# Attention inside a fused kernel: exponentials kept in PSUM, halves split before the transpose, one product for a pair's sinks

## The chip, the cores and the metric

The kernel runs on one core of a Trainium2 chip. The metric is the device time of one execution in microseconds; the time before is the median of three executions. One further execution was profiled, and all rows below come from it. PE is the matrix engine (PEld its weight loads), DVE the vector engine, ACT the scalar engine, POOL the general one, SP the engine whose queue issues most transfers.

## What is computed

Three stages, one after the other in the reference:

```python
# q, k, v: 4 batches, 8 heads, 768 positions, 64 wide; 4 sink keys, window of 128 keys
scores = scale * q @ k.T
scores = where(is_sink | in_window, scores, -1e9)
a = exp(scores - max(scores)); a = a / (sum(a) + 1e-9)
x = a @ v                                  # reshaped to 3072 tokens x 512
h = x @ w_in; x2 = (h - tanh(h)) @ w_out   # 512 -> 2048 -> 512
logits = x2 @ w_gate + modality_bias[id]   # 8 experts, the best one for each token
out = gate * (relu(x2 @ w1[e]) @ w2[e])    # only the chosen expert
```

## The kernel before

**Tiling.** The 3072 tokens are eight chunks of 384 tokens, three tiles of 128 each. Attention is cut into 192 units: a unit is one head and one tile of 128 queries, and its keys are at most 260 columns: the 128 of the tile before, 4 sinks, and the 128 of its own tile (132 columns where there is no tile before). Six units (two heads, three tiles) are a pair, so a chunk has four pairs, and there are 32 in all. Every product of 32-bit numbers is done as three products of 16-bit halves (low by high, high by low, high by high).

**A unit's way through the engines.** `scores` (L530): two products into a PSUM bank; DVE adds the mask and writes the negated result to `probs` in SBUF (L552) with the row's extreme; ACT takes the exponential from `probs` to `probs` (L557) and sums the row. `normalise` (L562): two tiny DVE operations invert the sum, and ACT writes `normed`, 128 by 260 numbers of 32 bits (L575). `transpose_probs` (L600): PE turns the two blocks of 128 columns (L611) into one of two PSUM banks used in turn, `pt_ps`; ACT copies them out as 16-bit high halves (L594), and DVE subtracts these from the PSUM to get the low halves (L598). Once a pair, DVE gathers the sink columns of six units (L586), PE turns them in three transposes (L625), and ACT and DVE split them in the same way. `weigh_values` (L629) multiplies the halves with those of the values; in a pair's last unit three more products of 384 columns weigh the sinks (L665). `split_x` (L676) copies the finished 384 columns out.

**Order of the work.** The order on each engine is written by hand. The first 28 units run by themselves (`alone`, L1191), beside the conversion of the weights. The others run inside the next chunk products: a `window` (L1208) is one chunk's 16 blocks of the 512-2048-512 stage, in 32 slots. An even slot holds the 12 products of 384 columns of `mlp_in` (L706) for the next block, an odd slot the 9 of 512 columns of `mlp_out` (L762). The slots of a list called `rest` have no unit; from the second window on these are 1, 4, 6, 7, 19, 20, 22 and 26. In a slot with unit n, PE does two thirds of the block's products, then

```python
stage(scores, E, eng, n)
stage(transposes, E, eng, n - 2)
```

then the remaining third, then `weigh_values` of unit n - 3. ACT's order in an even slot is: transposed halves of n - 2, `tanh` of the block (L718), `normalise` of n - 1, exponential of n. In an odd slot `mlp_split` (L737) stands in the place of `tanh`. DVE's order is: (odd slots) `mlp_gate` (L727); inversion of n - 1; mask of n; low halves of n - 2; (odd slots) `mlp_rest` (L747).

**The gate's products.** From the second window on, the chunk before is gated: `gate_slot` (L894), called ahead of everything else in a slot, puts on PE four transposes at slots 5, 11 and 17 (L796), the products for the logits at 7, 13 and 19 (L811), and two ranking products at 25 (L862). In windows 0, 2 and 4 a small product (`spread`, L311) stands at the head of slot 9. All of them borrow the bank of the scores, `s_ps`. Whoever writes to that bank first waits for whoever read it last (`claim_scores`, L670): after a unit's scores the reader is DVE's mask operation, which signals `shifted`.

**After attention.** In the last window the first expert's weights are loaded and prepared, and the experts' products follow.

## Time and profile before

| | |
|---|---|
| median of 3 runs | 1141.67 us (1139.27 to 1142.0) |
| the profiled execution's own time | 1141.86 us |
| its span | 1140.2 us |
| mean granted PE clock | 0.972 |
| units alone | about 15 to 92 us |
| windows 0 to 6, with units | about 92 to 735 us |
| window 7, then experts | 735 to 1140 us |

The span is the profile's first instruction to the last; the time holds 1.7 us more around it. Busy shares are averages over these stretches, and are read stretch by stretch.

### The profile page before, as it was taken

The page shows a single profiled execution, that of the slowest core. Times are in us where ns is not written, and L with a number is a line of the kernel's source. Part 1 is how long each engine was busy: PE and PEld are TensorE (multiplying, and loading weights), DVE is VectorE, ACT ScalarE, POOL GpSimd, SP SyncE. Part 2 cuts the span into 40 slices and gives each one's busy share as a digit, 9 for nine tenths or more (in the row PEclk, how much of TensorE's full clock was granted, in tenths as well). Part 3 has the DMA queues.
Part 4 walks back from the last instruction along what each step waited for, and adds up shares of the span by engine and source line. Part 5 has one row for each costly group of instructions (what it writes and reads, how often), then busy time and mean ns, then how long its engine had stood idle before and what let it go on. Part 6 is the DMA issues. An engine that isn't in the chain of part 4 may idle for free.

```text
span 1140.2 us, 24342 instructions
## 1 busy us (share of the span) xinstructions
PE 1017.1 (89%) x7840; PEld 664.2 (58%) x7840; DVE 729.6 (64%) x2388; ACT 618.5 (54%) x1421; POOL 397.3 (35%) x457
## 2 busy tenths in 40 slices
PE   1657888999999999999999999998896999789997
PEld 0534555565665665566566566654664677567774
DVE  6787978677977867887867876547563333443331
ACT  2675877575766766667666667445322222332221
POOL 3786876222345312325412321110122222122222
PEclk9976999999999999999999999999998999889999
DMA  9832111231212322311231130050023111001111
GB/s 284 282 97 53 34 34 34 75 109 34 61 37 63 62 90 58 69 35 34 38 90 34 34 61 2 1 203 2 29 79 136 43 46 56 28 23 52 46 46 45
DMA packets 24427, 75.14 MB, mean 66 GB/s; under 512 B 9680, under 2 KB 9808, under 8 KB 22800
## 3 DMA queue, kind: packets, MB, share of 16 engines
q1 hardware_dynamic: 15440, 60.58, 19.9%
q0 software_dynamic: 5728, 13.43, 3.8%
q8 instruction: 44, 0.72, 0.3%
q14 instruction: 47, 0.39, 0.1%
q10 hardware_dynamic: 3168, 0.02, 0.1%
HBM read 60.16 MB, written 14.12 MB: 65 GB/s over the span
## 4 chain that ended last, share of the span: by engine, by line
PE 67%; DVE 15%; ACT 6%; issue 6%; POOL 2%; DMA 2%; DVEq 0%; ACTq 0%; SPq 0%; POOLq 0%
PE h_ps L706 16%; PE acc L762 14%; PE pt_ps L1766 11%; PE h_ps L1817 6%; PE acc L1817 5%; PE x_out L665 4%; PE s_ps L542 2%; PE pt_ps L611 2%; DVE g_raw L727 2%; DVE qk_top L385 2%; DVE qk_exp L394 1%; PE s_ps L811 1%; DVE ew_lo L1478 1%; DVE g_lo L747 1%; ACT probs L557 1%
## 5 line engine op out<-in xcount | busy, mean ns | idle before, releaser
L762 PE MATMUL acc<-w_out_all,g_hi 128*128 128x512 f16 x768 | 228.3, 379 | 0.0
L706 PE MATMUL h_ps<-xt_hi,w_in_all 128*128 128x384 f16 x1024 | 211.1, 329 | 16.9 <-DVE g_raw L727 16.8
L762 PE MATMUL acc<-w_out_all,g_lo 128*128 128x512 f16 x384 | 145.4, 379 | 2.5 <-POOL w_out_all L350 1.2
L594 ACT ACTIVATE pt_hi<-pt_ps 128x256 f16<-128x256 f32 (+2 forms) x224 | 83.6, 380 | 110.0 <-PE pt_ps L611 106.0
L706 PEld LDWEIGHTS h_ps<-xt_hi,w_in_all 128*128 128x128 f16 x1024 | 97.6, 99 | 78.2 <-DVE g_raw L727 16.3
L98 POOL TENSOR_TENSOR tick<-tick 1x1 f32<-1x1 f32 x83 | 15.3, 184 | 313.0 <-ACT y L1833 97.8
L747 DVE SCALAR_TENSOR_TENSOR g_lo<-g_raw,batch_scale,g_hi 128x384 f16<-128x384 f32 x128 | 95.2, 743 | 33.1 <-ACT g_hi L737 30.7
L762 PEld LDWEIGHTS acc<-w_out_all,g_hi 128*128 128x128 f16 x768 | 75.0, 98 | 69.2
L598 DVE TENSOR_TENSOR pt_lo<-pt_ps,pt_hi 128x256 f16<-128x256 f32 (+2 forms) x224 | 94.3, 423 | 29.9 <-ACT pt_hi L594 28.2
L718 ACT ACTIVATE g_raw<-h_ps,batch_scale 128x384 f32<-128x384 f32 x128 | 74.3, 580 | 71.8 <-PE h_ps L706 70.5
L432 POOL TENSOR_TENSOR q_stack<-qk_raw,q_stack 64x768 f16<-64x768 f32 x31 | 50.8, 1639 | 165.5 <-ACT q_stack L428 165.5
L706 PE MATMUL h_ps<-xt_lo,w_in_all 128*128 128x384 f16 x512 | 106.1, 331 | 0.0
L575 ACT ACTIVATE normed<-probs,row_sum 128x260 f32<-128x260 f32 (+1 forms) x192 | 92.9, 484 | 21.1 <-DVE row_sum L570 20.9
L727 DVE SCALAR_TENSOR_TENSOR g_raw<-h_ps,batch_scale,g_raw 128x384 f32<-128x384 f32 x128 | 78.4, 612 | 37.9 <-ACT g_raw L718 36.5
L737 ACT ACTIVATE g_hi<-g_raw,batch_scale 128x384 f16<-128x384 f32 x128 | 78.0, 609 | 45.2 <-DVE g_raw L727 44.7
L1783 DVE SCALAR_TENSOR_TENSOR hid_lo<-pt_ps,hid_hi 128x512 f16<-128x512 f32 x50 | 34.6, 691 | 96.5 <-ACT hid_hi L1780 91.9
L557 ACT ACTIVATE probs<-probs,neg_max 128x260 f32<-128x260 f32 (+1 forms) x192 | 92.8, 483 | 5.8 <-DVE neg_max L552 5.7
L432 POOL TENSOR_TENSOR kl_stack<-qk_raw,kh_stack 128x1048 f16<-128x1048 f32 (+1 forms) x31 | 60.2, 1941 | 99.1 <-ACT kh_stack L428 98.4
L611 PE MATMUL pt_ps<-ident,normed 128*128 128x128 f32 x352 | 74.0, 286 | 22.7 <-ACT normed L575 22.6
L552 DVE CUSTOM_DVE_ANT_0 probs<-s_ps,mask 128x260 f32<-128x260 f32 (+1 forms) x180 | 73.1, 406 | 24.1 <-issue 22.9
L1766 PE MATMUL pt_ps<-xg_lo,ew_hi 128*128 128x128 f16 x800 | 79.0, 222 | 1.5 <-DVE xg_lo L1752 1.4
L409 POOL TENSOR_SCALAR qk_raw<-qk_raw,qk_scale 128x768 f32<-128x768 f32 (+2 forms) x62 | 61.0, 996 | 52.3 <-DVE qk_scale L400 52.3
(293 smaller groups left out, 2237.3 us busy)
## 6 DMA issues: line engine op xcount, KB each, us to landing
qk_raw<-in_qk SPq DMA_DIRECT2D x64, 454.0 KB, 6.1
raw<-in_w SPq DMA_DIRECT2D x16, 512.0 KB, 7.7
v_raw<-in_v SPq DMA_DIRECT2D x4, 1536.0 KB, 9.7
x_tokens<-x SPq DMA_DIRECT2D x24, 256.0 KB, 5.3
w_in_all<-in_w_in SPq DMA_DIRECT2D x4, 1024.0 KB, 13.2
w_out_all<-in_w_out SPq DMA_DIRECT2D x4, 1024.0 KB, 12.3
x_tokens<-g_raw SPq DMA_DIRECT2D x1, 1024.0 KB, 14.0
slots<-payload,dest POOLq DMA_INDIRECT x24
```

Source lines behind the costliest of these rows:

```text
L432: eng.tensor_tensor(lo, raw[half], hi[half], ALU.subtract).then_inc(q["conv_lo"], 1)
L557: eng.activation(probs[:, r, cols], probs[:, r, cols], ACT.Exp, bias=neg_max[:, r:r + 1], scale=-1.0, accum_out=row_sum[:, r:r + 1]).then_ ...
L575: eng.activation(normed[:, u % 6, cols], probs[:, r, cols], ACT.Copy, scale=row_sum[:, r:r + 1])\
L594: eng.activation(pt_hi[:, at, :], out, ACT.Copy).then_inc(q["pt_hi_done"], 1)
L598: eng.tensor_tensor(pt_lo[:, at, :], out, pt_hi[:, at, :], ALU.subtract).then_inc(q["pt_lo_done"], 1)
L611: mm = eng.transpose(out[:, b, :], normed[:, u % 6, b * KB:b * KB + P], ident[:])
L706: mm = eng.matmul(h_ps, w16[0][:, f, x * DM + k * P:x * DM + (k + 1) * P], r[:, par, k, :], start=(i == 0), stop=(i == 3 * KD - 1))
L727: eng.scalar_tensor_tensor(g, h_ps, batch_scale[:, b, 0:1], g, ALU.mult, ALU.subtract).then_inc(q["g_done"], 1)
L747: eng.scalar_tensor_tensor(g_lo[f % 2][:], g, batch_scale[:, b, 1:2], g_hi[f % 2][:], ALU.mult, ALU.subtract)\
L762: mm = eng.matmul(acc[t][:, :], l[f % 2][:, t * P:(t + 1) * P], w16[1][:, f, x * DM:(x + 1) * DM], start=(f == 0 and i == 0), stop=(f == N ...
L1766: mm = eng.matmul(hid_ps[c][:, (f - 4 * c) * P:(f - 4 * c + 1) * P], w[:, k, f * P:(f + 1) * P], x[p][:, k * P:(k + 1) * P], start=(i == 0 ...
L1817: mm = eng.matmul(y_ps[bank][:, :], l[:, f * P:(f + 1) * P], rhs, start=(f == 0 and i == 0), stop=(f == KF - 1 and i == 2))
```

## The change

Per unit:

- The scores of unit n go to `s_ps` for even n and to the second of the two former `pt_ps` banks for odd n. The mask operation is as before, but ACT writes the exponential over the scores, into that PSUM bank.
- ACT's `normalise` reads PSUM and writes the high half at once (`halves`, 16 bits). A new DVE operation, `normalise_rest`, multiplies the exponential in PSUM by the inverse sum, subtracts the high half, and writes the low half. It signals `normal_lo`, and stands where the low half of the transposed block stood, but for unit n - 1 where that was for n - 2.
- PE turns high and low halves apart: four 16-bit transposes for two 32-bit ones, into the one bank left for them. ACT copies all four blocks out in one operation of 512 columns; DVE has no part in that.
- A bank of the scores is free when `normal_lo` of its unit is signalled, where it was free at `shifted`. The gate's products and `spread` take the bank that the next unit will use (`free_bank`).

Per pair: the six units' sink columns are gathered in two DVE copies, high, low and high again, in 64 columns for each tile; three 16-bit transposes follow the unit's own under one signal; ACT copies 64 by 384 out; one product with the stacked value halves `vs` takes the place of three. For it the sinks' values are loaded to three places, six small transfers a batch instead of two.

```diff
         def scores(E, eng, a, u):
-            bank = acc[0] if a == 0 and u % 2 else s_bank
+            bank = score_bank[n % 2]
             if E == "pe":
-                if bank is s_bank:
-                    claim_scores(eng, (q["shifted"], n + 1))
-                else:
-                    need(eng, q["shifted"], n - 1)
+                claim_scores(eng, bank, (q["normal_lo"], n + 1))
...
-                eng.activation(probs[:, r, cols], probs[:, r, cols], ACT.Exp, bias=neg_max[:, r:r + 1],
+                eng.activation(bank[:, cols], probs[:, r, cols], ACT.Exp, bias=neg_max[:, r:r + 1],
                                scale=-1.0, accum_out=row_sum[:, r:r + 1]).then_inc(q["exped"], 1)
         def normalise(E, eng, a, u):
...
-                eng.activation(normed[:, u % 6, cols], probs[:, r, cols], ACT.Copy, scale=row_sum[:, r:r + 1])\
-                   .then_inc(q["normal"], 1)
+                eng.activation(half_of(u, 0, cols), score_bank[n % 2][:, cols], ACT.Copy, scale=row_sum[:, r:r + 1])\
+                   .then_inc(q["normal_hi"], 1)
+
+        def normalise_rest(E, eng, a, u):
...
+            if E == "dve":
+                eng.wait_ge(q["inverted"], 2 * n + 2)
+                eng.wait_ge(q["normal_hi"], n + 1)
+                eng.scalar_tensor_tensor(half_of(u, 1, cols), score_bank[n % 2][:, cols], row_sum[:, r:r + 1],
+                                         half_of(u, 0, cols), ALU.mult, ALU.subtract).then_inc(q["normal_lo"], 1)
         def transpose_probs(E, eng, a, u):
...
-                eng.wait_ge(q["normal"], n + 1)
-                need(eng, q["pt_lo_done"], m - 1)
-                for b in range(first, 2):
-                    mm = eng.transpose(out[:, b, :], normed[:, u % 6, b * KB:b * KB + P], ident[:])
+                eng.wait_ge(q["normal_lo"], n + 1)
+                need(eng, q["pt_done"], n)
+                need(eng, q["pts_done"], g)
+                for x in range(2):
+                    for b in range(first, 2):
+                        mm = eng.transpose(turned_probs[:, x, b, :], half_of(u, x, slice(b * KB, b * KB + P)), ident16[:])
+                if with_sinks:
+                    eng.wait_ge(q["sink_copied"], g + 1)
+                    for t in range(TPC):
+                        mm = eng.transpose(turned_sinks[:, t, :], sinks[:, t, :], ident16[:])
                 mm.then_inc(q["transposed"], 1)
...
+                eng.activation(pt[:, :, at, :], turned_probs[:, :, first:2, :], ACT.Copy).then_inc(q["pt_done"], 1)
         def weigh_values(E, eng, a, u):
...
                 if u % 6 == 5:
-                    for pt, values in ((pt_lo, vs_hi), (pt_hi, vs_lo), (pt_hi, vs_hi)):
-                        ops.append((x_out.rearrange("p (t c) -> p t c", t=TPC), values[par][:, hp * P:(hp + 1) * P],
-                                    pt[:, 12:12 + TPC, :]))
+                    ops.append((x_out, vs[par][0:SR, hp * P:(hp + 1) * P], pts[0:SR, :, :]))
...
-        def claim_scores(eng, *readers):
-            for sem_, count in score_readers:
+        def claim_scores(eng, bank, *readers):
+            for sem_, count in score_readers.get(bank is s_bank, ()):
                 need(eng, sem_, count)
-            score_readers[:] = readers
+            score_readers[bank is s_bank] = readers
...
                     stage(normalise, E, eng, n - 1)
                     stage(scores, E, eng, n)
-                    stage(transposes, E, eng, n - 2)
+                    stage(normalise_rest, E, eng, n - 1)
```

What moves on PE, at the head of slot 11 of window 1, from the scores of slot 10 to those of slot 11 (the names in brackets are the semaphores waited for; L796 and L818 are the gate's transposes). Before:

```order
L542 MATMUL s_ps<-kl_stack,q_stack 128x132 [waits f_shifted,f_conv_lo]
L542 MATMUL s_ps<-kh_stack,q_stack 128x132
L611 MATMUL pt_ps<-ident,normed 128x128 [waits f_pt_lo_done,f_normal]
L611 MATMUL pt_ps<-ident,normed 128x128
L706 MATMUL h_ps<-xt_hi,w_in_all 128x384 x4
L796 MATMUL s_ps<-ident,x_1 128x128 [waits f_shifted,f_evac_dve,f_evac_act]
L796 MATMUL s_ps<-ident,x_1 128x128 x3
L762 MATMUL acc<-w_out_all,g_lo 128x512 [waits f_g_lo_done]
```

and with the change, at the same place:

```order
L559 MATMUL s_ps<-kl_stack,q_stack 128x132 [waits f_normal_lo,f_conv_lo]
L559 MATMUL s_ps<-kh_stack,q_stack 128x132
L635 MATMUL pt_ps<-ident,halves 128x128 [waits f_pts_done,f_pt_done,f_normal_lo]
L635 MATMUL pt_ps<-ident,halves 128x128 x3
L728 MATMUL h_ps<-xt_hi,w_in_all 128x384 x4
L818 MATMUL pt_ps<-ident,x_1 128x128 [waits f_normal_lo,f_evac_dve,f_evac_act]
L818 MATMUL pt_ps<-ident,x_1 128x128 x3
L784 MATMUL acc<-w_out_all,g_lo 128x512 [waits f_g_lo_done]
```

No work has changed places on PE; the scores and the gate's transposes now wait for `f_normal_lo`, and so does everything that stands behind them.

What moves on DVE, in slots 10 and 11 of the same window, from the inversion for slot 10 to the gate operation of slot 11 (L551 to L552 and L568 to L569 are the mask operation). Before:

```order
L569 TENSOR_SCALAR row_sum<-row_sum 128x1 [waits f_exped]
L570 RECIPROCAL row_sum<-row_sum 128x1 [waits f_inverted]
L551 MEMSET tick 1x1 [waits f_normal,f_scores]
L552 ISA probs,neg_max<-s_ps,mask 128x132
L552 ISA neg_max 128x1
L598 TENSOR_TENSOR pt_lo<-pt_ps,pt_hi 128x256 [waits f_pv_done,f_pt_hi_done]
L586 COPY sinks<-normed 128x3x8 [waits f_normal,f_transposed]
L727 SCALAR_TENSOR_TENSOR g_raw<-h_ps,batch_scale,g_raw 128x384 [waits f_tanh_done]
```

and with the change:

```order
L590 TENSOR_SCALAR row_sum<-row_sum 128x1 [waits f_exped]
L591 RECIPROCAL row_sum<-row_sum 128x1 [waits f_inverted]
L568 MEMSET tick 1x1 [waits f_normal_lo,f_scores]
L569 ISA probs,neg_max<-s_ps,mask 128x132
L569 ISA neg_max 128x1
L607 SCALAR_TENSOR_TENSOR halves<-pt_ps,row_sum,halves 128x260 [waits f_normal_hi,f_inverted]
L618 COPY sinks<-halves 128x3x16 [waits f_normal_lo,f_transposed]
L619 COPY sinks<-halves 128x3x8
L749 SCALAR_TENSOR_TENSOR g_raw<-h_ps,batch_scale,g_raw 128x384 [waits f_tanh_done]
```

The operation ahead of the gate's (L749) now waits for ACT's `normalise` (`f_normal_hi`) instead of ACT's copy of transposed blocks, which stands two places earlier in ACT's order; the gather of sinks is two copies.

## Rows read from the trace of the kernel before

**Rows 1.** The page, part 1: busy time, share of the span, instructions.

```profile
PE 1017.1 (89%) x7840; PEld 664.2 (58%) x7840; DVE 729.6 (64%) x2388; ACT 618.5 (54%) x1421; POOL 397.3 (35%) x457
```

**Rows 2.** Stretches: bounds, length, engines' busy time (instructions), PE clock, DMA share, GB/s.

```profile
15.00:92.00 77.00, 43.67 (x328) 29.87 (x328) 61.30 (x240) 52.37 (x141) 59.27 (x58) 0.87 0.66 206
...
477.00:568.00 91.00, 87.34 (x578) 55.07 (x577) 73.56 (x254) 63.23 (x156) 37.41 (x33) 1.00 0.21 50
```

**Rows 3.** PE's waits in window 4 (477 to 568 us): total, times, longest.

```profile
PE s_ps L862 <- DVE neg_max L552: 1.3, 1, 1.3
PE s_ps L542 <- ACT x2t L801: 1.2, 2, 0.7
PE h_ps L706 <- DVE g_raw L727: 1.2, 2, 0.7
```

**Rows 4.** Groups by form, 205 to 735 us: busy, mean ns, idle before.

```profile
L575 ACT ACTIVATE normed<-probs,row_sum 128x260 f32<-128x260 f32 x117 | 58.6, 501 | 2.5 <-DVE row_sum L570 2.5
L727 DVE SCALAR_TENSOR_TENSOR g_raw<-h_ps,batch_scale,g_raw 128x384 f32<-128x384 f32 x95 | 58.1, 612 | 21.0 <-ACT g_raw L718 20.2
L598 DVE TENSOR_TENSOR pt_lo<-pt_ps,pt_hi 128x256 f16<-128x256 f32 x118 | 49.9, 423 | 15.0 <-ACT pt_hi L594 14.3
L594 ACT ACTIVATE pt_hi<-pt_ps 128x256 f16<-128x256 f32 x118 | 45.1, 382 | 89.1 <-PE pt_ps L611 88.3
L801 ACT ACTIVATE x2t<-s_ps 128x512 f32<-128x512 f32 x18 | 10.5, 584 | 0.0
```

**Rows 5.** Timeline, window 4, slots 10 and 11: start, length, engine, operation.

```profile
506.04 0.22 PE L665 MATMUL x_out<-pt_hi,v_hi 128*128 128x128 f16 x1
506.09 0.61 PE L796 MATMUL s_ps<-ident,x 128*128 128x128 f32 x4
506.13 0.58 ACT L718 ACTIVATE g_raw<-h_ps,batch_scale 128x384 f32<-128x384 f32 x1 [0.27 <-PE h_ps L706]
506.54 0.38 PE L762 MATMUL acc<-w_out_all,g_lo 128*128 128x512 f16 x1
506.61 0.50 ACT L575 ACTIVATE normed<-probs,row_sum 128x260 f32<-128x260 f32 x1
508.66 0.28 PE L542 MATMUL s_ps<-kl_stack,q_stack 128*128 128x260 f16 x1 [0.66 <-ACT x2t L801]
```

**Rows 6.** Timeline, window 3, slot 11, its scores.

```profile
417.50 0.28 PE L542 MATMUL s_ps<-kl_stack,q_stack 128*128 128x260 f16 x1 [0.21 <-ACT x2t L801]
```

**Rows 7.** Timeline, window 4, end of slot 18 and head of slot 19.

```profile
533.33 0.33 PE L665 MATMUL x_out<-pt_lo,vs_hi 128*128 128x384 f16 x1
...
533.49 0.33 PE L665 MATMUL x_out<-pt_hi,vs_lo 128*128 128x384 f16 x1
...
533.52 0.50 ACT L575 ACTIVATE normed<-probs,row_sum 128x260 f32<-128x260 f32 x1
...
533.82 0.95 PE L811 MATMUL s_ps<-w_gate,x2t 128*128 128x8 f32 x8
```

**Rows 8.** Timeline, window 4, head of slot 25.

```profile
549.72 0.51 ACT L575 ACTIVATE normed<-probs,row_sum 128x260 f32<-128x260 f32 x1 [0.69 <-DVE row_sum L570]
...
550.16 0.19 PE L862 MATMUL s_ps<-chosen,tri 128*128 128x24 bf16 x1 [1.26 <-DVE neg_max L552]
```

**Rows 9.** Timeline, window 6: an odd slot without gate work.

```profile
700.06 0.50 ACT L575 ACTIVATE normed<-probs,row_sum 128x260 f32<-128x260 f32 x1
...
701.00 0.27 PE L542 MATMUL s_ps<-kl_stack,q_stack 128*128 128x260 f16 x1
```

**Rows 10.** Timeline, units alone: ACT's `normed`, and DVE's next low half.

```profile
52.06 0.51 ACT L575 ACTIVATE normed<-probs,row_sum 128x260 f32<-128x260 f32 x1 [0.56 <-DVE row_sum L570]
...
52.36 0.28 DVE L598 TENSOR_TENSOR pt_lo<-pt_ps,pt_hi 128x128 f16<-128x128 f32 x1
```

**Rows 11.** Timeline, window 0: the longest wait of PE there.

```profile
151.87 1.44 PE L706 MATMUL h_ps<-xt_hi,w_in_all 128*128 128x384 f16 x4 [3.10 <-DVE g_raw L727]
```

**Rows 12.** Stretches: the four microseconds behind that wait.

```profile
152.00:156.00 4.00, 4.00 (x18) 2.26 (x17) 1.92 (x7) 1.52 (x3) 3.26 (x4) 0.60 0.82 191
```

184 lines of the change are left out of this document (98 added, 86 removed).

## The prediction

> **What bounds the kernel now.** I read four views. The page first: PE is busy for 89% of the span, the other engines for at most 64% [rows 1]. A share over the whole span says little here, so I cut it into stretches. While the first 28 units run alone, PE is busy for 44 of 77 us, and DVE for 61, ACT for 52 and POOL for 59: there no engine is full, they wait for each other. In window 4, which stands for the windows with units, PE is busy for 87.3 of 91 us at full clock, DVE for 73.6 and ACT for 63.2 [rows 2]. The third view, PE's waits in that window, comes to 3.7 us [rows 3]. So a window is as long as PE's work, and what the change is worth there is the work it takes from PE less the new waits it gives to PE. The fourth view, the timeline of single slots, shows how close those waits are.
>
> **PE's work.** A 32-bit transpose takes 0.11 us (four from 506.09 to 506.54), a 16-bit product of 128 columns 0.05 us (from 506.04 to the next start) [rows 5]. Two of the former make 0.22 us, four of the latter 0.20 to 0.22: the unit's transposes are worth nothing. A pair's three sink transposes save 3 x 0.06 = 0.17 us. A product of 384 columns takes 0.16 us [rows 7], and two fall away: 0.32 us. Windows 1 to 6 hold 138 units, 23 pairs: 3.9 us from the transposes, and from the products 7.4 us, of which I count only 11 of 23 pairs, 3.5 us, since the other 12 stand right ahead of a new wait that swallows them (below). **Term 1: -7.4 us.**
>
> **When a bank of the scores is free.** Before, it was free with the mask operation, the first thing DVE does with the scores. Now it is free with the low half, which comes after the exponential, the inversion and ACT's high half. In unit numbers: in the slot of unit n-1, ACT does the high half of n-2 and DVE its low half; the bank is wanted again in the slot of n. In an even slot ACT does `tanh` ahead of that high half, and `tanh` waits for the end of PE's whole block of that slot. So the low half of n-2 cannot be ready until PE has ended the block, `tanh` (0.58 us) and the high half have run, and DVE has followed. All that PE has left in the slot by then is `weigh_values`. In window 4 `tanh` starts at 506.13 and `normed` ends at 507.11 [rows 5].
>
> How long is the low half? No row has a 260-column operation with a scale from a pointer that reads PSUM and 16 bits. Below it lies the 256-column subtraction, 0.42 us, above it the 384-column operation of the same kind, 0.61 us [rows 4]. I take 0.53, near the middle and meant to hold the two hand-overs (ACT to DVE, DVE to PE).
>
> The high half lies between 0.38 us (256 columns out of PSUM without a pointer) and 0.50 us (260 columns with one, out of SBUF) [rows 4]; I take 0.50, the row with the same operands but for the source. The Trainium skill (ScalarE: Activation LUTs, the tip on PSUM in "Step-by-step: what each stage is for") calls PSUM the lower-latency side for an ACTIVATE's destination. It would speak for faster exponentials, which write to PSUM now; by it the sum would be somewhat less than by the row. If the gain were as large as the whole distance of the two rows, 0.12 us at each of the 60 places counted below, the sum would be 7 us less.
>
> **The gate's products are the first to want the bank.** They stand at the head of a slot, ahead of the chunk products, so they meet the wait in full. Slots 11, 13, 17, 19 and 25 (9 in windows 0, 2, 4) follow an even slot with a unit.
> - Transposes, slots 11 and 17 of six windows, 12 places: `normed` ends at 507.11, the low half at 507.64, and PE was there at 506.09: 1.55 us late [rows 5]. In return PE's wait for `x2t` at the same slot's scores shrinks, 0.66 us in windows 2 and 4 [rows 5], 0.21 us in others [rows 6]. 4 x 0.89 + 8 x 1.34 = 14.3 us.
> - Logits, slots 13 and 19, 12 places: 533.52 + 0.50 + 0.53 = 534.55 against 533.82 [rows 7]: 0.73 us each, 8.8 us. The slot before holds the sinks' products, and PE's time saved there only makes PE arrive earlier at this wait.
> - Ranking, slot 25, 6 places: 549.72 + 0.51 + 0.53 = 550.76 against 550.16 [rows 8]: 0.60 us on top of the wait that is there, 3.6 us.
> - `spread`, 3 places: between the logits' 0.73 and the transposes' 1.55; I take 1.2, since no sinks delay PE ahead of it: 3.6 us.
>
> Queued behind each of these on PE is the slot's whole block, and behind that everything. **Term 2: +30.3 us** (23 to 36).
>
> **The scores themselves** stand behind two thirds of a block and arrive later. In an odd slot without gate work `normed` ends at 700.56, so the low half at 701.09, and PE is there at 701.00 [rows 9]: 0.09 us, at 27 places (slots 3, 15, 29, 31, and 9 in odd windows): **Term 3: +2.4 us** (0 to 6). The unit's transposes stand behind and wait for the same signal, so they add nothing.
>
> **ACT's longer copy** goes from 256 to 512 columns, 0.38 to 0.58 us [rows 4]: +0.20 us a unit. In the windows I cost it at nothing: ACT sits idle for 89 us ahead of these copies in 530 us [rows 4], and in even slots it waits 0.27 us more between the copy and `tanh` [rows 5]. Without that cover it would be 138 x 0.20 = 28 us. DVE's sum hardly changes: 0.53 for 0.42 us a unit, less a 384-column subtraction and plus a small copy a pair. But it waits longer for ACT, and `g_lo` is late by about half a microsecond in odd slots; its reader is PE's next odd slot, two slots on, and DVE is 17 us short of full [rows 2].
>
> **Units alone, and window 0.** There ACT's `normed` ended at 52.57, 0.21 us after DVE had begun its low half of the unit before [rows 10]; now DVE has to wait that out, and its own operation is some 0.1 us longer. 28 x 0.3 = 8.4 us if DVE were always the one that is late; if none of it is on the path, nothing. Scores no longer run ahead either: they wait for the low half, which ties PE, ACT and DVE into one round. I take 6 us, and 2 us for the 26 units of window 0, where the conversion of the weights holds up much anyway. **Term 4: +8 us** (0 to 20). The four more small transfers a batch and the new constants I count at nothing: the DMA engines' share is 0.21 in window 4 [rows 2], and the constants are made before the first keys are there.
>
> **Sum.** -7.4 + 30.3 + 2.4 + 8 = +33.3 us. The profiled execution took 1141.9 us, 0.2 us above the median, so either gives 1175 us. The low ends give 1141.9 - 7.4 + 23 = 1157, the high ends 1141.9 - 7.4 + 36 + 6 + 20 = 1197.
>
> **Rivals.**
> - *The waits are covered and PE's saving counts* (faster). PE would save 23 x 0.49 = 11 us: 1131 us. It needs the low half 1.55 us earlier in slots 11 and 17, that is ahead of `tanh` on ACT. ACT's order speaks against it: the high half stands behind `tanh`. From there on it decides: if the waits come to less than 11 us in all. Chance 0.10.
> - *The new waits take the place of old ones*: while PE waits, DVE and ACT catch up, and the 3.7 us of window 4 [rows 3] vanish in each of six windows. I have taken 4 us of that with the `x2t` waits already; the other 18 would leave 1157 us, and with nothing lost in the units alone 1149. For: `g_raw` is late where DVE was held up. Against: PE's wait for the bank delays the scores that DVE waits for. Down to 1145 us chance 0.08; within 0.3% 0.05.
> - *The clock falls in the new waits.* After a wait of 3.10 us [rows 11] the granted clock was 0.60 over the next 4 us, a mean of stretches at 2.4 and 1.2 GHz [rows 12], which costs some 1.6 us. If that came at each of the 33 places of term 2, it would be 53 us more: 1228 us. Against it: window 4 has a wait of 1.26 us [rows 8] and is at 1.00 throughout [rows 2], and the new waits are near that length. The Trainium skill (TensorE: Matmul & The Clock Gate, "HAM oscillation — how this bites in real kernels") says that idle gaps between bursts of matmuls bring the clock back to half; the trace agrees for the 3.10 us, and not for 1.26. Chance 0.04.
> - *The units alone become one long round*: term 4 at its high end or above, 1187 to 1200 us. Chance 0.10, nearly all of it in the range.
>
> **How the numbers follow.** The forecast as summed, 1157 to 1187 us, has 0.63; with the others that makes 0.85 for slower. A change of 0.3% (3.4 us) is about what a measurement of this kernel can tell from none. The range 1148 to 1198 leaves out the faster and the equal case (0.15), a little between 1145 and 1148, and the clock.
>
> **What would show it.** Right: in the profile after, PE waits for the low half (L607) ahead of L818, L833 and L884, by some 1.5, 1.0 and 2 us, about 5 us more waiting in each of windows 1 to 6, which grow from 91 to about 95 us; PE's busy time is less; the low half takes 0.43 to 0.53 us, the copy 0.58 us. Wrong: windows of 91 us or less; PE waits that name `x2t` or `g_raw` instead; a clock below 1.00 in them; or units alone that end well before 92 us, which would mean that the exponentials in PSUM shorten the round.

## The result, and the profile after

The changed kernel takes 1225.49 us (median of 4 runs, 1223.54 to 1228.47) against 1141.46 us in the same comparison: a ratio of 1.0755, 95% interval 1.0734 to 1.0777 (the two medians alone divide to 1.074). The direction was forecast, the size was not: +84 us for +33. The profiled execution spans 1222.5 us.

To see where the time went I cut both traces at the same four points: the starts of PE's scores of unit 0, of unit 28 (window 0 begins), of unit 54 (window 1) and of unit 191, the last. All numbers called "stages" below are distances between these starts, read from the timelines, in us; the last runs to the end of the span:

```
                 alone   window 0   windows 1-6   after unit 191
before            90.6    101.2       517.9          414.7
after             97.7    110.1       580.1          418.5
difference        +7.1     +8.9       +62.2           +3.8
forecast            +6     +3.2         +24              0
```

(The forecast's +3.2 in window 0 is its 2 us and one `spread`; +24 is the rest of terms 1 to 3.) The windows hold three quarters of the loss. The first stage ends only with the first scores of window 0: from unit 0 to unit 27, the last that runs alone, it is 75.1 us before and 86.7 after. So the units alone lost 11.6 us, of which 4.5 vanish in the wait for window 0. PE's part 1 of the page now reads, against [rows 1]:

```profile
PE 1040.2 (85%) x8128; PEld 654.0 (53%) x8128; DVE 693.7 (57%) x2388; ACT 651.2 (53%) x1421; POOL 395.4 (32%) x459
```

and two stretches, one with the units alone and one in the windows (columns as in [rows 2]):

```profile
15.00:98.00 83.00, 44.19 (x347) 31.56 (x347) 56.49 (x232) 53.88 (x134) 57.62 (x56) 0.76 0.61 192
...
530.00:630.00 100.00, 88.01 (x605) 51.80 (x603) 68.08 (x251) 64.91 (x150) 37.59 (x34) 1.00 0.18 39
```

In the windows PE is busy for 88 of 100 us where it was busy for 96 of 100 [rows 2], and in this stretch the clock stays at 1.00. In windows 1 to 6 as a whole it fell once, to 1.2 GHz, in slot 11 of window 1 (0.50 over 254.0 to 256.8 us). Here is that slot, from the scores of slot 10 to its own, then the same slot of window 3 (columns as in [rows 2]), and the wait of PE in each:

```profile
250.38:256.52 6.14, 4.42 (x20) 2.22 (x21) 2.39 (x12) 2.53 (x6) 0.00 (x0) 0.75 0.24 97
454.90:459.54 4.64, 2.92 (x21) 1.71 (x21) 2.39 (x12) 2.53 (x6) 0.00 (x0) 1.00 0.32 130
```

```profile
253.26 0.91 PE L818 MATMUL pt_ps<-ident,x 128*128 128x128 f32 x4 [1.72 <-DVE halves L607]
457.78 0.63 PE L818 MATMUL pt_ps<-ident,x 128*128 128x128 f32 x4 [1.73 <-DVE halves L607]
```

So the rival with a falling clock had the price of one fall about right, 1.5 us for 1.6, but it came at one place and not at 33; that its 1228 us lies near the measured time is chance. In windows 1 to 6 of the profiled executions the clock never fell in the kernel before, e1, e5, e13, b2, h1 and h2; it fell once in the change, e8 and e10, twice in e12, three times in e2, e3, e7 and e9, four times in e4 and e11, and five times in e6. Where two runs differ in this, "at equal clock" below is my estimate from the slots in which it fell, up to 1.5 us each.

PE's waits from 224 to 804 us (windows 1 to 6; total, times, longest), to be held against [rows 3]:

```profile
PE pt_ps L818 <- DVE halves L607: 19.7, 12, 1.7
PE pt_ps L833 <- DVE halves L607: 10.5, 12, 0.9
PE s_ps L884 <- DVE halves L607: 9.3, 5, 1.9
PE h_ps L728 <- DVE g_raw L749: 7.9, 13, 1.1
PE s_ps L559 <- DVE halves L607: 3.6, 17, 0.2
PE pt_ps L332 <- DVE halves L607: 3.0, 2, 1.7
```

The same units before, from 208 to 726 us:

```profile
PE s_ps L862 <- DVE neg_max L552: 5.4, 5, 1.3
PE h_ps L706 <- DVE g_raw L727: 5.3, 10, 0.8
PE s_ps L542 <- ACT x2t L801: 3.1, 7, 0.7
```

The waits of the first list are the waits that were forecast, at the places that were forecast, for the low half (L607). Slots 10 and 11 of window 4, the place of [rows 5], show the chain as it was foretold: `tanh`, the high half, the low half, and PE waiting 1.55 us at the gate's transposes.

```profile
558.48 0.22 PE L687 MATMUL x_out<-pt,v_hi 128*128 128x128 f16 x1
...
558.57 0.58 ACT L740 ACTIVATE g_raw<-h_ps,batch_scale 128x384 f32<-128x384 f32 x1
559.05 0.47 ACT L596 ACTIVATE halves<-pt_ps,row_sum 128x260 f16<-128x260 f32 x1
...
559.62 0.49 DVE L607 SCALAR_TENSOR_TENSOR halves<-pt_ps,row_sum,halves 128x260 f16<-128x260 f32 x1 [1.32 <-ACT halves L596]
...
560.25 0.63 PE L818 MATMUL pt_ps<-ident,x 128*128 128x128 f32 x4 [1.55 <-DVE halves L607]
```

The prediction worked out 1.55 us too, but from start to start. From start to start it is 1.72 us here, since PE could have begun at 558.53, 0.05 us behind the start of its last product, and the view counts from that product's end at 558.70. That the two figures are alike is luck. What slots 11 and 17 grew by is the fair comparison: 0.92 us in windows 2 and 4 for a forecast of 0.89, and 1.44 to 1.57 in the others for 1.34 (leaving out the slot with the fallen clock).

But the 54 us of waits in the first list, with 14 us before and a saving of 7 us to come off, do not make +62. Part of the rest does not show as waiting. PE's whole time in these windows, before and after (columns as in [rows 2]):

```profile
207.66:725.52 517.86, 503.44 (x3305) 316.18 (x3303) 396.49 (x1407) 347.93 (x871) 162.91 (x134) 1.00 0.23 52
223.84:803.99 580.15, 517.99 (x3510) 303.03 (x3509) 370.49 (x1404) 369.89 (x871) 161.59 (x134) 1.00 0.20 47
```

PE was idle for 14 us and is idle for 62; its busy time should have fallen by 7 us and rose by 14.6. In the slot above, the first 0.17 us of the wait count as busy (1.72 less 1.55); for the 54 waits that are new this is an estimated 9 us.

Cut by slot (the mean growth of the interval that ends at a slot's scores, windows 1 to 6), the gate's slots grew by 1.57 (11), 0.93 (13), 1.32 (17), 0.93 (21, behind the logits of 19), 0.75 (25), and 1.93 and 1.58 (the two `spread`s in 9): 35.8 us in all, 1.5 of it the clock's, for some 29 forecast there. The other slots grew by 26.5 us, even ones as much as odd ones (10: 0.27, 12: 0.27, 14: 0.29, 15: 0.26, 16: 0.30, 18: 0.24), the most 30 (0.62), 27 (0.54) and 2 (0.51), where I had -5. The chain of work through windows 1 to 6 shows what sort of loss that is (share of each line), first before (208 to 726 us), then after (224 to 804 us):

```profile
by line: PE h_ps L706 27.7%; PE acc L762 25.9%; PE x_out L665 7.9%; PE s_ps L542 4.7%; PE pt_ps L611 4.3%; issue 4.2%; PE s_ps L811 2.7%; DVE qk_top L385 1.9%; DVE g_lo L747 1.8%; DVE g_raw L727 1.7%; DVE qk_exp L394 1.6%; PE pt_ps L625 1.5
```

```profile
by line: PE acc L784 18.6%; PE h_ps L728 18.0%; issue 12.1%; ACT halves L596 7.4%; DVE halves L607 6.7%; PE pt_ps L635 3.5%; DVE qk_top L406 3.0%; DVE g_raw L749 2.7%; PE s_ps L559 2.6%; ACT g_hi L759 2.3%; PE pt_ps L833 2.2%; PE x_out L687
```

PE's two kinds of chunk products held 54% of the chain and hold 37%; the two halves, which were not on it, hold 14%. The windows are no longer as long as PE's work. DVE's waits in the same two stretches say the same: it stood 13.2 us for ACT's copy ahead of its low half before, and stands 135.5 us for ACT's high half now (first line before, second after):

```profile
DVE pt_lo L598 <- ACT pt_hi L594: 13.2, 63, 0.3
```

```profile
DVE halves L607 <- ACT halves L596: 135.5, 129, 2.0
```

The single durations were forecast well: low half 0.49 us for 0.53, high half 0.47 for 0.50, copy 0.60 for 0.58 (groups by form, 224 to 804 us):

```profile
L646 ACT ACTIVATE pt<-pt_ps 128x512 f16<-128x512 f16 x115 | 68.6, 596 | 118.7 <-PE pt_ps L635 79.5 <-PE pt_ps L639 38.3
L607 DVE SCALAR_TENSOR_TENSOR halves<-pt_ps,row_sum,halves 128x260 f16<-128x260 f32 x58 | 28.4, 489 | 57.6 <-ACT halves L596 57.6
L596 ACT ACTIVATE halves<-pt_ps,row_sum 128x260 f16<-128x260 f32 x58 | 27.3, 471 | 0.0
```

### The profile page after: what moved, and what is told of

It is laid out like the page before. It is cut to its first block, busy times and chain, and to the rows that moved or that the text cites. A ratio compares the mean times of both kernels' runs of the same rounds, so it can differ in the third digit from the quotient of the medians.

```text
span 1222.5 us, 24886 instructions
## 1 busy us (share of the span) xinstructions
PE 1040.2 (85%) x8128; PEld 654.0 (53%) x8128; DVE 693.7 (57%) x2388; ACT 651.2 (53%) x1421; POOL 395.4 (32%) x459
## 4 chain that ended last, share of the span: by engine, by line
PE 42%; issue 19%; DVE 18%; ACT 11%; DMA 4%; POOL 4%; POOLq 1%; ACTq 0%; DVEq 0%; SPq 0%
PE h_ps L728 12%; PE acc L784 11%; ACT halves L596 5%; PE pt_ps L1789 4%; DVE halves L607 4%; DMA slot_g<-slots 2%; PE pt_ps L635 2%; DVE qk_top L406 2%; DVE g_raw L749 2%; PE h_ps L1840 2%; PE acc L1840 2%; PE s_ps L559 2%; ACT g_hi L759 2%; PE x_out L687 1%; POOL xg L1733 1%
## 5 line engine op out<-in xcount | busy, mean ns | idle before, releaser
L646 ACT ACTIVATE pt<-pt_ps 128x512 f16<-128x512 f16 (+1 forms) x192 | 107.4, 559 | 155.2 <-PE pt_ps L635 104.3
L728 PEld LDWEIGHTS h_ps<-xt_hi,w_in_all 128*128 128x128 f16 x1024 | 92.6, 98 | 84.4 <-DVE g_raw L749 19.2
L769 DVE SCALAR_TENSOR_TENSOR g_lo<-g_raw,batch_scale,g_hi 128x384 f16<-128x384 f32 x128 | 82.5, 644 | 31.0 <-ACT g_hi L759 30.8
L607 DVE SCALAR_TENSOR_TENSOR halves<-s_ps,row_sum,halves 128x260 f16<-128x260 f32 (+1 forms) x96 | 44.7, 466 | 95.0 <-ACT halves L596 94.5
L687 PE MATMUL x_out<-pt,v_hi 128*128 128x128 f16 (+1 forms) x448 | 88.5, 260 | 10.7 <-issue 5.8
L607 DVE SCALAR_TENSOR_TENSOR halves<-pt_ps,row_sum,halves 128x260 f16<-128x260 f32 (+1 forms) x96 | 44.8, 466 | 92.0 <-ACT halves L596 91.2
L749 DVE SCALAR_TENSOR_TENSOR g_raw<-h_ps,batch_scale,g_raw 128x384 f32<-128x384 f32 x128 | 78.4, 612 | 30.3 <-ACT g_raw L740 28.9
L1789 PE MATMUL pt_ps<-xg_hi,ew_lo 128*128 128x128 f16 x800 | 79.8, 224 | 0.0
L1789 PE MATMUL pt_ps<-xg_hi,ew_hi 128*128 128x128 f16 x800 | 79.5, 223 | 0.0
```

The source lines that it names most:

```text
L607: eng.scalar_tensor_tensor(half_of(u, 1, cols), score_bank[n % 2][:, cols], row_sum[:, r:r + 1], half_of(u, 0, cols), ALU.mult, ALU.subtra ...
L646: eng.activation(pt[:, :, at, :], turned_probs[:, :, first:2, :], ACT.Copy).then_inc(q["pt_done"], 1)
L687: mm = eng.matmul(o, l, r, start=(begins and i == 0), stop=(u % 6 == 5 and i == len(ops) - 1), skip_group_check=True)
L728: mm = eng.matmul(h_ps, w16[0][:, f, x * DM + k * P:x * DM + (k + 1) * P], r[:, par, k, :], start=(i == 0), stop=(i == 3 * KD - 1))
L749: eng.scalar_tensor_tensor(g, h_ps, batch_scale[:, b, 0:1], g, ALU.mult, ALU.subtract).then_inc(q["g_done"], 1)
L769: eng.scalar_tensor_tensor(g_lo[f % 2][:], g, batch_scale[:, b, 1:2], g_hi[f % 2][:], ALU.mult, ALU.subtract)\
```

## The experiments

Theory A: the low half, behind ACT's high half, behind `tanh`, is late for everything that wants a bank, in all slots. Theory B: what is late are the transposes, which need both halves wherever the exponential stands. Theory C: ACT's and DVE's work is the round, and PE's waits only show it. Ratios are against the kernel before, with 95% intervals; stages are given where they tell more.

**e1: the exponential back in SBUF, the bank free with the mask operation.**

```
-  claim_scores(eng, bank, (q["normal_lo"], n + 1))
+  claim_scores(eng, bank, (q["shifted"], n + 1))
-  eng.activation(bank[:, cols], probs[:, r, cols], ACT.Exp, ...)
+  eng.activation(probs[:, r, cols], probs[:, r, cols], ACT.Exp, ...)
   (high and low half read probs[:, r, cols] too)
```

> The change with one part undone: the exponential goes to SBUF again, ACT's high half and DVE's low half read it there, and a bank of the scores is free with the mask operation. The 16-bit halves, their transposes, the single copy out and the single sinks product stay. Theory A (the late bank is what costs): the waits for the low half ahead of the gate's products (L818, L833, L884) and ahead of the scores go, 36 us of gate slots and most of the 27 us of the ordinary slots; with PE's saving of up to 11 us coming out and the units alone about 5 us shorter than in the change, 1225.5 less 65 to 85 us: 1140 to 1160. Theory B (the two halves in a row cost, wherever the exponential stands: the transposes, which follow the scores, wait for the low half too, and ACT's copy is longer): only the gate's waits go, the ordinary slots keep their 27 us: 1180 to 1192.

1203.1 us, ratio 1.056 (1.053 to 1.059): neither. Windows 1 to 6 take 550.0 us, 30 less than in the change, and the waits ahead of the gate's products are gone; but +32 against before stay, with PE now waiting at the transposes (L635) and for the gate's readers. The units alone take 106.7 us, 9 more than in the change (5 of it from unit 0 to unit 27). A reason is in the low half itself. POOL and DVE, 70.3 to 72 us:

```profile
70.43 1.15 POOL L371 TENSOR_TENSOR w_in_all<-w_in_all 128x512 f16<-128x512 f32 x1
70.54 1.33 DVE L607 SCALAR_TENSOR_TENSOR halves<-probs,row_sum,halves 128x260 f16<-128x260 f32 x1 [0.36 <-ACT halves L596]
```

It takes 1.33 us for 0.49 and ends 0.29 us after POOL's operation does. With both inputs in SBUF it takes up to 2.42 us; with the scores' side in PSUM, as in the change, none of 192 takes more than 0.49. So this run undid one cost and made another, and it bounds the bank's share from below only. In windows 1 to 6 the new cost is small: 22 of 138 low halves took over 0.60 us, and all that they took over 0.49 comes to 6.5 us. Most of the +32 there has another cause.

**e2, e8, e9: ACT's high half first** in all slots of the windows, in the even ones alone, in the odd ones alone. Of e2 (e8 has the first hunk, e9 the second):

```
   if even:
+      stage(normalise, E, eng, n - 1)
       stage(transposes, E, eng, n - 2)
       mlp_in(E, eng, *nxt)                # tanh
-      stage(normalise, E, eng, n - 1)
   else:
+      stage(normalise, E, eng, n - 1)
       stage(transposes, E, eng, n - 2)
       mlp_split(E, eng, *nxt)             # g_hi
-      stage(normalise, E, eng, n - 1)
```

> The change with ACT's order alone altered: in every slot of the windows the high half stands ahead of the copy and of tanh or g_hi, instead of behind them. Nothing is left out. Theory A (the low half is late because ACT's high half stands behind the copy and tanh, and the bank waits for it): the high half comes 0.5 to 1.2 us earlier, the waits ahead of L818 and L833 shrink to under 0.6 us, and the ordinary slots' 0.2 us vanish: 1165 to 1190. Theory C (ACT's and DVE's work as such is the round, whatever its order, or PE is slower for another reason): within 8 us of 1225.

1181.9 us, ratio 1.037 (1.034 to 1.040): theory A. Windows 1 to 6 take 542.6 us, 37.5 less, though the clock fell three times in them for once in the change.

> The change with ACT's high half ahead of the copy and of tanh in the even slots alone; odd slots as in the change. Theory A (each slot's order shows at the bank one slot on): the waits that go are those of the odd slots, the gate's 5.6 us a window down to some 2 and the odd slots' scores (3, 15, 31) 0.5 us: 3 to 4 us a window, some 20 to 27 us in all, 1198 to 1205; the even slots' scores still wait 0.2 to 0.4 us each. Rival (the round of two slots is full, so that time won in one half is lost in the other): under 10 us.

1186.1 us, ratio 1.042 (1.039 to 1.044), better than expected. Windows 1 to 6 take 546.1 us, 34.0 less: nearly all of it. PE's waits for the low half at the logits (L833, 10.5 us) and `spread` (L332, 3.0) are gone, at the transposes 7.6 us stay for 19.7, at the ranking all (222.4 to 768.5 us, its windows 1 to 6):

```profile
PE s_ps L884 <- DVE halves L607: 9.3, 5, 1.9
PE pt_ps L818 <- DVE halves L607: 7.6, 12, 1.1
PE h_ps L728 <- DVE g_raw L749: 5.5, 11, 0.7
PE s_ps L559 <- DVE halves L607: 2.5, 12, 0.2
```

The gate's slots keep some 8 of their 35.8 us; the even slots' scores wait as in the change.

> The change with ACT's high half ahead of the copy and of g_hi in the odd slots alone; even slots as in the change. Theory A: what goes are the waits of the even slots' scores (0, 10, 12, 14, 16, 18, 24 and 28: 2.2 us a window), which my prediction had at nothing, so 13 us in windows 1 to 6 and some in window 0: 1207 to 1213. What the prediction implies (the even slots' scores come after the bank is free, so nothing is to be had): 1222 to 1228.

1229.3 us, ratio 1.080 (1.077 to 1.083): nothing won. This is the run that corrected my theory. The even slots' scores do come earlier, as I expected (their slots grew by 0.12 in 10, 0.06 in 12, 0.00 in 14, 0.10 in 16 where the change had 0.27 to 0.30), but the time comes back in slot 2 (1.26 for 0.51), 25 (1.69 for 0.75) and 31 (0.81 for 0.26). PE waits longer there, for `g_raw` (11.1 us for 7.9) and at the ranking (11.8 for 9.3). Windows 1 to 6 take 583.2 us for 580.1; at equal clock they are level. So the even slots' waits are real, and mending them alone wins nothing: something else ends last. Behind e8's edit the same edit does count, since e2, which has both, is 3.5 us shorter in the windows.

**e3: ACT copies the transposed high halves alone.** The low half of the probabilities is left out of the result. The gate then chooses other experts, and what follows unit 191 grows by 78 us: only stages can be compared.

```
-  eng.activation(pt[:, :, at, :], turned_probs[:, :, first:2, :], ACT.Copy)
+  eng.activation(pt[:, 0, at, :], turned_probs[:, 0, first:2, :], ACT.Copy)
-  for x, values in ((1, v_hi), (0, v_lo), (0, v_hi)):
+  for x, values in ((0, v_hi), (0, v_lo), (0, v_hi)):
```

> The change, but ACT copies only the transposed high halves out, 256 columns in place of 512 (0.38 us for 0.60), and the products that read the transposed low halves read the high ones instead, as many and as long: the low half of the probabilities is left out of the result. Theory A (ACT's longer copy stands ahead of g_hi and of the high half in odd slots, and ahead of tanh and the high half in even ones, on the way to the bank): some 0.15 us in each of the 138 ordinary units, 20 us, and some of the gate's waits: 1195 to 1208. My prediction's reading (the copy is covered by ACT's idle time): 1222 to 1227.

1296.7 us as a whole. The copy takes 0.384 us for 0.596:

```profile
L646 ACT ACTIVATE pt<-pt_ps 128x256 f16<-128x256 f16 x116 | 44.5, 384 | 122.0 <-PE pt_ps L635 84.7 <-PE pt_ps L639 36.5
```

Windows 1 to 6 take 576.1 us, 4.0 less for 138 shorter copies, some 7 less at equal clock; without any cover it would have been 28. The prediction's reading held in the main, ACT's idle time covers most of the longer copy; theory A's 20 us were wrong.

**e5: the gate's products behind the first third of their block.**

```
   for t in range(TPC):
       ...
+      if t == 0 and early:
+          early()                         # before_slot(E, eng, w, k)
       if t == 1 and between:
           between()
```

> The change with the gate's products and spread moved in PE's order from the head of their odd slots to behind the first third of the block (the first of three t of mlp_out), 0.95 us later; ACT and DVE keep their order. Nothing is left out. Theory A (the wait ahead of them is a loss of its own, since PE has other work that needs no bank): the transposes' 1.57 us shrinks by about 0.95, the logits' 0.9 and the ranking's 0.75 go nearly whole: 12 x 0.95 + 12 x 0.85 + 6 x 0.75 + 3 x 0.95, 29 us less, 1196; half of it if the scores then wait for the gate's readers, 1211. Theory C (the round of ACT and DVE sets the windows, and the waits only show it): 1220 to 1228.

1211.5 us, ratio 1.064 (1.061 to 1.066): the lower of theory A's two numbers. Windows 1 to 6 win 14.3 us of some 28 (1.5 of it the clock's); the transposes still wait (11.9 us for 19.7), and in slots 11 and 25 the scores now wait for the gate's readers instead.

**e4: PE's saving given back**: two more products a pair, on zeros.

```
+  ops += 2 * [(x_out, vs[par][0:SR, ...], nil[0:SR, :, :])]
   ops.append((x_out, vs[par][0:SR, ...], pts[0:SR, :, :]))
```

> The change with two more products a pair ahead of the single one for the sinks, of the same 384 columns and the same weights, on a tile of zeros (it adds nothing to the sums): PE gets back the 0.32 us a pair that the change took from it. If PE's saving is swallowed by the wait for the low half that follows (the ordinary slots wait as well as the gate's): 0 to 4 us over the change, 1225 to 1229. My prediction's term (11 of 23 pairs in the windows count): some 4 to 5 us, 1230. If it all counts: 32 x 0.32, 10 us, 1235.

1232.4 us, ratio 1.083 (1.080 to 1.085), 7 us over the change. Windows 1 to 6 take 588.2 us, 8.1 more, but that is not 0.35 for each of 23 pairs. Cut by slot, 3.9 us stand in slots 5 and 29, where 9 of the 11 pairs cost 0.32 or 0.33 us each. In slots 13 and 21, where a wait of the gate's products for the low half follows, 10 of the 12 pairs cost nothing (0.01 us or less). The other 4.1 us stand in slots in which the clock fell. Work added to PE counts where no such wait stands right behind it, and is swallowed where one does: the prediction's term.

**e6, e7: DVE's low half ahead of the next mask operation**, in the windows, then with both orders for the units alone as well.

```
   stage(normalise, E, eng, n - 1)
+  stage(normalise_rest, E, eng, n - 1)
   stage(scores, E, eng, n)
-  stage(normalise_rest, E, eng, n - 1)
```

> The run with ACT's high half first in the slot (1182 us), and on DVE the low half ahead of the mask operation of the next unit in the windows, instead of behind it. Nothing is left out. What is left of the waits in that run is the low half ahead of the ranking (2.5 us in slot 25) and the transposes (1.1 us in slot 17), and there DVE does the mask operation, which waits for PE's scores at two thirds of the block, before the low half. Theory A: those go, 1.2 us in slot 25, 0.7 in 17 and about 0.5 in 16, 24 and 31: 15 us less, 1164 to 1172. Rival (DVE then waits for ACT's high half ahead of the mask operation, so the exponentials are later and the loss only moves): 1178 or more.

1191.8 us, ratio 1.046 (1.044 to 1.048): the rival, 10 us worse than e2. In windows 1 to 6, where 3 of the 9 us lost are the clock's, DVE waits 86.4 us for the high half where it waited 16.4 in e2, with the mask operation behind it.

> The run before it (high half first on ACT, low half ahead of the mask operation on DVE, in the windows), with the same two orders for the 28 units that run alone. Theory A: there DVE stands 23 us waiting for ACT's high half behind the copy, and the stretch is 7 us longer than before; with the high half first 4 to 8 us of it come back, against the run without it. Rival (the stretch is longer because its gaps bring the granted clock to 0.73, and for the weights' conversion): within 2 us.

1195.6 us, ratio 1.049 (1.046 to 1.051); the units alone take 103.5 us for 100.0. From unit 0 to unit 27 it is 87.1 us for 88.7, and 86.6 to 88.7 in the runs that leave this part as it is in the change. No gain; the order is not what makes them long.

**b2: a control**, e2's edit in the kernel before.

> The kernel before, with ACT's normalisation ahead of the copies and of tanh or g_hi in the windows: the same order as in the second run. A control: if that order is worth something by itself, whatever the change, the kernel before gains too, up to its 18 us of waits in windows 1 to 6: 1120 to 1135. If what it mended there was made by the change (before, PE wanted only normed, two slots later): 1136 to 1146.

1151.6 us, ratio 1.011 (1.009 to 1.012): 1% slower. The order that mends the change hurts the kernel before, so it is not a gain of its own that e2 shows.

**e10: e2 and e5 together.**

> Both orders together: ACT's high half first in every slot of the windows (1182 us alone) and the gate's products behind the first third of their block (14 us less alone). Theory A (what is left of the gate's waits with the high half first is 2.5 us in slot 25, 1.1 in slot 17 and 0.3 in slot 11, and 0.95 us of each is lateness of the low half): 8 to 14 us less, 1168 to 1174. Rival (the ranking of slot 25 waits for the gate's choice on DVE, and ACT and DVE stand waiting for the gate's products instead): 1178 or more. Either way still above the kernel before, since the units alone and window 0 keep 13 us.

1180.2 us, ratio 1.037 (1.034 to 1.039). The rival: 2 us less in the windows than e2, which the clock explains (one fall for three). The gate's transposes wait 2.4 us in all, and nothing follows from it.

**h1, h2: the kernel before with the sinks' part alone**, on 64 rows as in the change, then on 128. DVE halves the gathered sinks, PE transposes them as 16-bit numbers, DVE copies them out, and one product takes the place of three. Of h2 against h1:

```
-  sinks = sb("sinks", [P, TPC, SR], F16)
+  sinks = sb("sinks", [P, TPC, P], F16)
-  ops.append((x_out, vs[par][0:SR, ...], pts[0:SR, :, :]))
+  ops.append((x_out, vs[par][:, ...], pts[:, :, :]))
```

> The kernel before with the sinks' part of the change alone: the gathered sinks are halved into 16 bits by DVE, transposed as 16-bit numbers, copied out by one DVE operation, and one product a pair takes the place of three; exponentials, normalisation and the other transposes are as before. Theory A (the last run but four showed 0.32 us a pair of products to count in full, and the sinks' transposes and DVE's shorter operation come on top): 23 x 0.32 to 23 x 0.49, 7 to 11 us less in the windows: 1128 to 1133. Rival (DVE's three small operations a pair and the later copy delay g_lo, or PE waits for the sinks): 1137 or more.

1145.8 us, ratio 1.006 (1.004 to 1.008): the rival's side, but not for its reasons. Slot 3 of window 4, PE, from the last products of the unit to the next block (start, length); first before, then h1, then h2:

```profile
487.43 0.33 PE L665 MATMUL x_out<-pt_hi,v_hi 128*128 128x256 f16 x2
487.60 0.33 PE L665 MATMUL x_out<-pt_lo,vs_hi 128*128 128x384 f16 x1
487.76 0.33 PE L665 MATMUL x_out<-pt_hi,vs_lo 128*128 128x384 f16 x1
487.92 0.33 PE L665 MATMUL x_out<-pt_hi,vs_hi 128*128 128x384 f16 x1
488.08 0.81 PE L706 MATMUL h_ps<-xt_hi,w_in_all 128*128 128x384 f16 x4
```

```profile
490.36 0.33 PE L678 MATMUL x_out<-pt_hi,v_hi 128*128 128x256 f16 x2
490.62 0.33 PE L678 MATMUL x_out<-pts,vs 64*128 64x384 f16 x1
490.88 0.82 PE L719 MATMUL h_ps<-xt_hi,w_in_all 128*128 128x384 f16 x4
```

```profile
481.20 0.33 PE L678 MATMUL x_out<-pt_hi,v_hi 128*128 128x256 f16 x2
481.36 0.33 PE L678 MATMUL x_out<-pts,vs 128*128 128x384 f16 x1
481.52 0.81 PE L719 MATMUL h_ps<-xt_hi,w_in_all 128*128 128x384 f16 x4
```

From the unit's last products to the next block it is 0.65 us before, 0.52 with one product on 64 rows and 0.32 with one on 128. The one on 64 rows starts 0.10 us late, and the block behind it 0.10 us late again. It saves 0.13 of the 0.33 us. The transposes into 64 rows save nothing: slots 3, 12, 18 and 28, which hold them, are 0.06 us longer than before.

> The kernel before with the sinks' part of the change alone, as in the run of it with 64 rows (1145.8, 0.6% slower than before), but on 128 rows. Theory A (the 64-row product cost 0.2 us a pair, of 32 pairs): 4 to 6 us less than that run, 1139 to 1142, level with the kernel before or a little under it in the windows. Rival (the slower time comes from DVE's three small operations a pair and from PE's wait for them): 1144 to 1148.

1131.8 us, ratio 0.993 (0.991 to 0.995): better than expected, and **the fastest version here, 0.7% faster than the kernel before**. Windows 1 to 6 take 509.0 us for 517.9, 0.39 us for each of 23 pairs; the slots behind the single product (5, 13, 21, 29) are 0.33 us shorter, those of the transposes (3, 12, 18, 28) 0.16, which are the prediction's two numbers, 0.32 and 0.17. Slot 2 takes 0.34 more in h1 and h2 alike; the cause of that stays open.

**e11: the change with the sinks on 128 rows.**

> The change with the sinks' operands widened from 64 to 128 rows: the gathered tile has 128 columns (zeros behind the first 64), so that transposes, copy and the single product use all 128 partitions, as the products around it do. Nothing is left out. In the change the product on 64 rows starts 0.10 us later than a 128-row one would, and the next instruction 0.27 us after it in place of 0.16, so the single product saves 0.11 us a pair, not 0.32; two more of them cost 0.33 for the two. Theory A (a change of the row count between products costs 0.1 us on each side): 0.2 us a pair, 4 to 7 us less: 1218 to 1222. Rival (the 0.2 us is a wait for the sinks' copy, late because it stands behind the unit's copy on ACT): no gain, 1223 to 1228.

1225.0 us, ratio 1.074 (1.071 to 1.076): the same as the change, and for neither reason. Slots 5 and 29 are 0.21 us shorter at all 11 places, 3 and 28 some 0.10; 13 and 21 are as they were, and slot 30 gives 0.21 back. At equal clock windows 1 to 6 would be some 3 us shorter. They take 581.3 us for 580.1, since the clock fell four times for once: that is what stands in slots 17 (1.80 for 1.32), 25 and 27. Of the six runs, the one with the highest mean clock (0.966) took 1218.2 us, the others (0.950 to 0.959) 1223.7 to 1226.7. Time taken from PE is worth something in the change, and less than the clock moves.

**e12: three banks for the first 24 units.**

```
+  def bank_of(n):
+      return (s_bank, pt_bank[1], acc[0])[n % 3] if n < UPC else score_bank[n % 2]
```

> The change with three banks for the scores of the first 24 units in place of two (acc of t = 0, which is free there, is the third), so that scores wait for the low half of three units back, not two. Windows as in the change. Theory A (the units alone are 7 us longer because PE waits 32 us for the low half at the scores): the scores' waits go and the stretch takes 90 to 93 us for 97.7, 4 to 7 us less. Rival (the transposes, which stand right behind the scores, wait for the low half of two units back anyway, and the round of ACT and DVE is what is long): within 1.5 us, with the waits now at the transposes (L635).

1223.6 us, ratio 1.074 (1.071 to 1.076): the rival. The units alone take 96.9 us for 97.7 (86.1 for 86.7 from unit 0 to unit 27). PE's waits there (16 to 110 us) only move, from the scores (15.9 and 15.8 us at L559 in the change) to the transposes:

```profile
PE pt_ps L635 <- DVE halves L607: 27.0, 18, 3.6
```

**e13: e2, e5, e11 and e12 together.**

> The change with all that helped or is expected to: ACT's high half first in the windows, the gate's products behind the first third, the sinks on 128 rows, three banks for the units alone. If the parts add up: 1180 less 5 for the rows, and less 0 to 6 for the banks, 1169 to 1176. The kernel before stays ahead of it by some 30 us, since what is left (13 us in the units alone and window 0, 20 us in the windows) is DVE and ACT standing in wait for each other.

1170.3 us, ratio 1.028 (1.025 to 1.030), as expected: windows 1 to 6 take 531.1 us, 13 more than before with 9 us less of work for PE. There the 128 rows count at every pair (slots 13 and 21 are 0.32 us shorter than before), and the windows are 9.6 us shorter than in e10, 1.7 of it the clock's: with the high half first, PE's time is partly the bound again.

## Why the prediction came out short, step by step

- **The gate's products wait for the low half (term 2): right in mechanism and place, 7 us short in size.** 35.8 us measured in the windows for 29, of which 1.5 are the clock's. That the high half's place behind the copy and `tanh` is the cause is shown by e8: with it ahead of both in the even slots 34.0 us go, 28 of them in the gate's slots, and b2 shows that the order has no worth of its own. No run moves it ahead of `tanh` alone; e3 shows that the copy's length has little part in it.
- **"So a window is as long as PE's work" is the step that failed**, and with it the sum's form, PE's work plus new waits at 60 places. The slots without the gate's products stood in the sum at -5 us (term 3 less term 1) and grew by 26.5: 31 of the 49 us by which the stages exceed the forecast. It was true of the kernel before: there PE is idle for 14 of 518 us, and where h2 takes 0.33 and 0.16 us from PE, the slots shrink by just that. In the change PE is idle for 62 of 580 us, and an earlier bank in half the slots (e9) is worth nothing, since PE then waits elsewhere. My reading is that ACT and DVE now wait for each other in every unit, because the low half needs the high half, and the next exponential's inversion stands on DVE behind the low half. DVE's 135.5 us of waits in place of 13.2 fit it, but it is argued and not shown: in e2 those waits are down to 16.4 us, and the windows are still 25 us longer than before. I read DVE's 17 us short of full in window 4 as room; DVE had no waits of this kind in its queue then.
- **Even slots' scores (term 3 counted odd slots alone, and 27 places for 25: slots 29 and 31 of window 6 have no unit).** That they wait was put at nothing without a row. They wait as the odd ones do, 0.24 to 0.30 us in slots 10 to 18. e9 shows that the 26.5 us of the ordinary slots do not go with these waits alone.
- **Term 1, -7.4 us: wrong in the size, right in the count.** One product on 64 rows saves 0.13 us, not 0.32, and the transposes into 64 rows cost 0.06 us in place of saving 0.17 (h1, h2). That 11 of 23 pairs count and 12 are swallowed at the gate's wait is what e4 and e11 show.
- **ACT's longer copy at nothing: right in the main.** In e3 the shorter copy wins 4 us in the windows, some 7 at equal clock, where no cover would have meant 28.
- **Term 4.** The units alone cost 11.6 us for 6, up to unit 27; 7.1 of them reach window 0. e12 shows that it is not the number of banks, e7 that it is not the order; the halves' row (exponential, inversion, high half, low half, transposes) is what remains, argued and not shown. The granted clock fell with PE's longer waits there, from 0.85 to 0.76 over 15 to 98 us. Window 0 cost 8.9 for 3.2, as I take it for the windows' reasons, which I had not thought to hold there; no run separates it. The 3.8 us behind unit 191 were put at nothing; the code there hardly differs, and it took 414.9 to 418.2 us in the other runs but e3, so a part of them may be chance.
- **The signs.** PE's waits ahead of L818, L833 and L884 and the lengths of the operations came out as named. But a window grew from 89 to 92 us to 99 to 104, not to 95, PE's busy time rose, and the clock fell once in the windows, which I had named as a sign of being wrong.
- **What stays open** is what holds the 13 us that e13 still has over the kernel before in windows 1 to 6. Neither the bank (e1), nor the copy (e3), nor DVE's order (e6), nor the gate's place (e10) settled it alone.

## What to carry to other kernels

Before pricing new waits against the engine that is full, ask whether that engine will still be the bound: an operation added in a row between two other engines (here ACT, then DVE, then the bank) can make a round of its own. Time taken from or given to the full engine then counts only where no wait stands right behind it, so price every slot in which the buffer is wanted, not only those that want it first. And before two runs are compared for a few us, see that the granted clock was the same in the stretch. A buffer's release is part of such a row: where a bank is freed three operations later, look at what stands ahead of each of them on its engine, and try moving the first one up before anything else (34 of the 62 us here, e8). A part of a change that is good by itself (one product for three) is best taken alone, and tried at full row count.

## What the runs showed of the hardware that was not expected

- **A product on 64 rows among products on 128** costs about 0.1 us on entering and 0.1 on leaving: 0.52 us where 128 rows take 0.32 (h1, h2), although it has half the rows; three transposes into 64 rows cost 0.22 us more than into 128 (slots 3, 12, 18 and 28 of h1 and h2); two more products on 64 rows behind the first cost 0.165 us each (e4). The Trainium skill (TensorEngine Tiling (Array Packing), "Key Properties") says that changing the tiling mode drains the engine; the trace agrees if a product on 64 rows counts as another mode.
- **DVE's operation with both inputs in SBUF is held by POOL's.** In e1 the low half took up to 2.42 us, and whenever it took over 0.7 us, an operation of POOL was under way, and it ended 0.1 to 0.3 us behind one; from PSUM, in the change, it took at most 0.49 us in all 192 cases. The Trainium skill (SBUF — State Buffer, "SBUF: two separate sides") describes an exclusive lock between a DVE operation with two SBUF inputs and a GpSimd operation that reads SBUF, held for the whole instruction; the trace agrees. That is what keeping the exponentials in PSUM was seen to save.
- **Where the exponential and its readers lie** matters little on ACT: 0.47 to 0.48 us with a side in PSUM (after), 0.505 with both in SBUF (e1).
- **The same wait does not always cost the clock.** In the change PE waited 1.72 us ahead of the gate's transposes in window 1 and 1.73 in window 3; behind the first the clock fell to 1.2 GHz and the slot took 1.5 us more, behind the second it stayed at 2.4.
